# Scores of a whole tile as two matmuls in tiles of 64 rows by 128 columns of TensorE, in place of four in tiles of 64 by 64

## The chip, the cores and the metric

The kernel runs on one core of one Trainium2 chip. The metric is the device time of one execution in microseconds. Engines are named as in the profile: PE is TensorE (PEld its weight loads), DVE is VectorE, ACT is ScalarE, POOL is GpSimd, SP is SyncE, which issues the DMAs.

## What is computed

Attention over 4 batches, 8 heads, 576 positions and 64 values per head, where each query keeps its 32 largest scores; behind it two feed-forward stages on the 2304 x 512 result. All inputs and outputs are f32. The reference, cut:

```python
scores = scale * np.matmul(q, k.transpose(0, 1, 3, 2))          # 4 x 8 x 576 x 576
kth = np.partition(scores, -top_k, axis=-1)[..., -top_k:-top_k + 1]
scores = np.where(scores >= kth, scores, -1000000000.0)
attn = softmax of scores                                        # written out in the reference
attn_out = np.matmul(attn, v)                                   # -> x: 2304 x 512

h = x @ w_in                                                    # 512 -> 2048
x = (h * (1.0 / (1.0 + np.exp(-1.702 * h)))) @ w_out            # 2048 -> 512

h = (x @ w1) * (x @ w2) @ w3                                    # 512 -> 1024 -> 1024
out = h @ w_out2                                                # 1024 -> 512
```

## The kernel before

**Tiles and chunks.** The 2304 tokens are cut into eight chunks of 288 (`CHUNK`), two to a batch. A chunk has 18 tiles of attention work (`CT`): for each of two groups of four heads (`g`) there are eight whole tiles of 128 queries of one head (two parts `t.j` of four heads), and ahead of them one leftover tile (`t.left`) that holds the last 32 queries of the four heads, 4 x 32 = 128 rows. In all that is 144 tiles, 128 whole ones and 16 leftover ones. A tile is a matrix of 128 queries by 576 scores.

**One slot, one tile.** Each engine has its own program, all written as a list of slots, one for each tile, by `run_chunks` and a function `step`. The order within a slot is written out by hand. PE's slot (lines 750 to 774) has: `scores` of the tile two slots ahead (L616), `transpose_probs` of a tile four slots back (L630, five transposes of 128 x 128), then three or four feed-forward units of 12 matmuls each with 288 moving columns of f16 (L702), and, every other slot, `weigh_values` of a pair of tiles (L661). In the first slots PE also spreads peaks of the weights over the partitions (`spread_peaks`, L672, one to three matmuls with an f32 stationary operand of 128 x 128) and multiplies w3 by w_out2 (`weight_product`, L694).

**The scores.** `qx` holds the queries and `kx` the keys of a group, both transposed: 64 values of a head on the partitions. SP loads both a second time into the other 64 partitions (`both_halves`), so that partitions 0 to 63 work on the first 288 keys (`half` 0) and partitions 64 to 127 on the other 288 (`half` 1). The results of the two halves go to two banks of PSUM, `ps[:, half, 0:288]`. A matmul (line 616) takes 64 rows of the array, from row `half * 64` on, and as many columns as it has queries; `tile_position` says which. In a whole tile the 128 queries are taken in two parts of 64, which gives four matmuls in four tiles of 64 by 64 of the array. In a leftover tile the four heads have 32 queries each, which gives eight matmuls in tiles of 64 by 32. The last of them signals `qk_done`. Stationary is the slice of queries, moving are 288 columns of keys.

**What waits for the scores.** PE itself waits ahead of them for `s_copied`, ACT's copy of the tile before out of PSUM (L790), since there is one pair of banks. ACT copies the tile, DVE searches its 32 largest values (L975 to L995, seven passes over three slots), POOL scales the edges (L1199), ACT makes the penalty (L801), POOL subtracts it (L1191), ACT takes the exponentials (L810), DVE and POOL invert and apply the sum (L1003, L1216), and then come the transposes and ACT's copy of them (L819). The feed-forward units pass through ACT (tanh L864, g_high L877), DVE (gate L1010) and POOL (g_low L1227) meanwhile. At the end of each chunk DVE also finds a peak (L1097).

**The stretches.** Up to about 310 us DVE, ACT and POOL also read the weights, find their peaks and split them into two f16 parts; from there on the same 18 slots repeat for each chunk until 970 us, and behind 970 us only feed-forward work is left.

Of the kernel before, what the change touches and what calls it, by code (L numbers as in the profile page):

```python
# [12 lines left out]
B, H, S, D = 4, 8, 576, 64  # L13
TOKENS, DM, FF1, FF2 = B * S, H * D, 2048, 1024
TOP_K = 32
P = 128
# [4 lines left out]
HG = 4  # L21
# [216 lines left out]
def wait_alone(eng, sem, value, passed):  # L238


    wait(eng, sem, value)
    if not isinstance(value, int):
        eng.sem_inc(passed, 1)
# [19 lines left out]
def build(nc, q_in, k_in, v_in, w_in_d, w_out_d, w1_d, w2_d, w3t_d, wo2_d, out_d, wx_d, w3o_d):  # L263
# [160 lines left out]
    with nc.Block() as block:  # L424
# [171 lines left out]
        def _(pe):  # L596
            def scores(t):

                if not t.exists():
                    return  # L600
                if t.left:

                    pe.wait_ge(q_loaded[t.g], t.chunk.count(32, 32))
                    pe.wait_ge(k_loaded[t.g], t.chunk.batch_count(32, 32))

                wait_alone(pe, s_copied, t.count(), passed_pe)
                if t.left:
                    parts = [(i, slice(FULL, CHUNK), i * LEFT) for i in range(HG)]
                else:
                    first = t.j * P  # L610
                    parts = [(t.h % HG, slice(first + c, first + c + D), c) for c in (0, D)]
                for i, queries, col in parts:
                    for half in range(2):

                        rows = slice(half * D, (half + 1) * D)
                        last = nc.tensor.matmul(ps[col:col + queries.stop - queries.start, half, 0:HALF],  # L616
                                                qx[rows, t.g, i, queries],
                                                kx[rows, t.g, i, half * HALF:(half + 1) * HALF],
                                                start=True, stop=True, tile_position=(half * D, col))
                last.then_inc(qk_done, 1)  # L620
# [129 lines left out]
            def step(chunk):  # L750
                for slot in slots(chunk):
                    at = slot.at()
                    product = at - WPROD_FIRST if at is not None else -1
                    units = units_in(slot)
                    scores(slot.next(2))
                    transpose_probs(slot.next(-4))
                    if at == V_SCALE_SLOT:
                        spread_peaks(0, 1, 0)
                    if at == W_SCALE_SLOT:
                        spread_peaks(1, 2, slot.next(-6).group_count())  # L760
                    if at == SECOND_SCALE_SLOT:
                        spread_peaks(2, 3, slot.next(-6).group_count())
                    spread_for = period_at(slot, X2_SPREAD)
                    if spread_for is not None:
                        spread_x2(spread_for)
                    for u in units[:1]:
                        unit(u)
                    if 0 <= product < 2 * WBLK:
                        weight_product(2 * product)
                    for u in units[1:]:  # L770
                        unit(u)
                    if 0 <= product < 2 * WBLK:
                        weight_product(2 * product + 1)
                    weigh_values(slot.next(-4))
# [509 lines left out]
```

## Time and profile before

| | us |
|---|---|
| median of 3 runs | 1141.3 |
| lowest, highest | 1140.41, 1143.19 |
| the profiled execution | 1140.66 |
| its span, from the first to the last instruction | 1138.9 |
| PE busy | 1043.7 |
| DVE busy | 877.6 |
| ACT busy | 675.0 |
| POOL busy | 566.4 |

An f32 matmul stands in the trace as two records, and so does its weight load. Busy time counts an engine's time with at least one instruction under way; matmuls overlap, so their durations don't add up to it. The records of PE's matmuls have modelled ends: the distance of two starts says more than the end of one. Times of the timeline and of the chain count from the start of the span.

### The profile page before, as it was taken

What the parts mean: (1) busy time and instruction counts of PE and PEld (TensorE: products, weight loads), DVE (VectorE), ACT (ScalarE), POOL (GpSimd) and SP (SyncE); (2) the same over time, 40 slices, a digit from 0 to 9 for tenths busy, and PEclk for the clock granted to TensorE, in tenths of its full rate; (3) what the DMA queues carried; (4) which work ended last, traced back from release to release, by engine and by line L of the source; (5) the groups of instructions that cost most, each with busy time, mean ns of one, the idle gap of its engine ahead of it and who ended that gap; (6) DMA issues with size and microseconds to landing.
All of it is one profiled execution on the core that took longest, in us unless ns stands there. A gap on an engine that the chain in (4) does not pass through costs nothing.

```text
span 1138.9 us, 27527 instructions
## 1 busy us (share of the span) xinstructions
PE 1043.7 (92%) x9452; PEld 754.4 (66%) x9452; DVE 877.6 (77%) x1970; ACT 675.0 (59%) x1346; POOL 566.4 (50%) x806
## 2 busy tenths in 40 slices
PE   2499878697799999999999999999999999999989
PEld 0244456465577777777677767777777767887767
DVE  5999998987798789877998789978987899422010
ACT  2358888877866467645765576546755676444112
POOL 1334678876775346543654356534753475413001
PEclk9999989788999999999999999999999999999999
DMA  9963632574444051433032232503140304033144
GB/s 292 374 222 112 182 99 79 145 203 148 149 148 118 2 147 40 134 73 117 23 113 59 68 93 81 155 29 111 47 126 1 96 20 122 10 96 94 56 142 141
DMA packets 63471, 127.14 MB, mean 112 GB/s; under 512 B 5728, under 2 KB 22624, under 8 KB 61536
## 3 DMA queue, kind: packets, MB, share of 16 engines
q1 hardware_dynamic: 63328, 125.33, 37.3%
q8 instruction: 78, 1.28, 0.5%
q14 instruction: 65, 0.53, 0.2%
HBM read 112.20 MB, written 13.11 MB: 110 GB/s over the span
## 4 chain that ended last, share of the span: by engine, by line
PE 66%; DVE 12%; issue 8%; POOL 7%; ACT 4%; DMA 2%; SPq 1%; DVEq 0%; POOLq 0%; ACTq 0%
PE ff_ps L702 48%; PE x_T_ps L661 7%; PE probs_T_ps L630 6%; PE scores_ps L616 5%; DVE peaks L1026 2%; POOL scores L1191 2%; DMA v_three_quarters<-v_rows_in 2%; POOL g_low L1227 2%; DVE search L992 1%; DVE top L983 1%; DVE top L975 1%; DVE search L986 1%; DVE search L980 1%; POOL piece_split L1231 1%; POOL scores L1216 1%
## 5 line engine op out<-in xcount | busy, mean ns | idle before, releaser
L1191 POOL TENSOR_TENSOR scores<-scores,penalty 128x576 f32<-128x576 f32 x144 | 203.1, 1410 | 111.7 <-ACT penalty L801 111.6
L702 PE MATMUL ff_ps<-x_high,w_ring 128*128 128x288 f16 x1024 | 195.9, 288 | 3.8 <-DVE x_low L1124 3.8
L819 ACT ACTIVATE probs_T<-probs_T_ps 128x640 f32<-128x640 f32 x144 | 100.9, 700 | 109.3 <-PE probs_T_ps L630 108.6
L801 ACT ACTIVATE penalty<-scores,edges 128x576 f32<-128x576 f32 x144 | 111.2, 772 | 83.6 <-POOL edges L1199 81.6
L702 PE MATMUL ff_ps<-x_T_high,w_in_high 128*128 128x288 f16 x512 | 149.2, 291 | 10.6 <-DVE gate L1010 10.2
L702 PE MATMUL ff_ps<-x_T_low,w_in_high 128*128 128x288 f16 x512 | 148.9, 291 | 0.0
L702 PE MATMUL ff_ps<-x_T_high,w_in_low 128*128 128x288 f16 x512 | 148.7, 290 | 0.0
L702 PE MATMUL ff_ps<-g_high,w_out_high 128*128 128x288 f16 x512 | 147.6, 288 | 0.0
L702 PE MATMUL ff_ps<-g_low,w_out_high 128*128 128x288 f16 x512 | 147.5, 288 | 0.0
L702 PE MATMUL ff_ps<-g_high,w_out_low 128*128 128x288 f16 x512 | 147.5, 288 | 0.0
L702 PE MATMUL ff_ps<-x_low,w_ring 128*128 128x288 f16 x512 | 147.4, 288 | 0.0
L630 PEld LDWEIGHTS probs_T_ps<-identity,scores 128*128 128x128 f32 x720 | 79.5, 145 | 92.6 <-issue 52.2
L616 PE MATMUL scores_ps<-keys,queries 64*64 64x288 f32 (+1 forms) x1280 | 110.4, 452 | 32.9 <-ACT scores L790 18.6
L630 PE MATMUL probs_T_ps<-identity,scores 128*128 128x128 f32 x720 | 114.7, 292 | 26.4 <-POOL scores L1216 26.4
L1227 POOL TENSOR_TENSOR g_low<-gate,g_high 128x288 f16<-128x288 f32 x128 | 92.8, 732 | 71.2 <-ACT g_high L877 70.5
L661 PE MATMUL x_T_ps<-probs_T,v_rows 128*64 128x128 f32 (+1 forms) x1920 | 110.9, 267 | 14.2 <-ACT probs_T L819 6.9
L1216 POOL TENSOR_SCALAR scores<-scores,inverse_total 128x576 f32<-128x576 f32 x144 | 107.7, 748 | 31.8 <-DVE inverse_total L1003 31.7
L975 DVE MAX8 top<-scores 128x8 f32<-128x576 f32 x144 | 108.1, 751 | 15.8 <-ACT scores L790 13.8
L702 PEld LDWEIGHTS ff_ps<-x_high,w_ring 128*128 128x128 f16 x1024 | 100.6, 98 | 29.0 <-issue 3.9
L661 PEld LDWEIGHTS x_T_ps<-probs_T,v_rows 128*64 128x64 f32 x1920 | 93.5, 144 | 38.2 <-issue 38.2
L1227 POOL TENSOR_TENSOR ab_low<-gate,ab_high 128x288 f16<-128x288 f32 x64 | 46.8, 732 | 139.8 <-ACT ab_high L886 139.8
L810 ACT ACTIVATE scores<-scores,edges 128x576 f32<-128x576 f32 x144 | 111.4, 774 | 4.4 <-POOL scores L1191 4.1
(90 smaller groups left out, 2178.5 us busy)
## 6 DMA issues: line engine op xcount, KB each, us to landing
w_ring<-second_weights SPq DMA_DIRECT2D x192, 256.0 KB, 2.6
queries<-q_T SPq DMA_DIRECT2D x32, 288.0 KB, 4.5
keys<-k_T SPq DMA_DIRECT2D x16, 576.0 KB, 8.5
second_weights<-piece_split SPq DMA_DIRECT2D x24, 256.0 KB, 4.4
out<-y_out SPq DMA_DIRECT2D x32, 144.0 KB, 2.9
v_rows<-v_rows_in SPq DMA_DIRECT2D x8, 512.0 KB, 4.2
w_T<-w_T_in SPq DMA_DIRECT2D x1, 4096.0 KB, 39.9
whole_weight<-w_in SPq DMA_DIRECT2D x2, 2048.0 KB, 16.9
```

What stands on the lines that cost most here:

```text
L616: last = nc.tensor.matmul(ps[col:col + queries.stop - queries.start, half, 0:HALF], qx[rows, t.g, i, queries], kx[rows, t.g, i, half * HAL ...
L630: last = nc.tensor.transpose(ptp[:, j * P:(j + 1) * P], row[:, min(j * P, S - P):min((j + 1) * P, S)], ident[:, :])
L661: last = nc.tensor.matmul(xq[odd * D:(odd + 1) * D, cols], vn[:, j, first:first + D], pt[:, tile.ring(2), j * P + queries.start:j * P + qu ...
L702: last = nc.tensor.matmul(out, stationary[i], moving[j], start=first and n == 0, stop=last_one and n == 2)
L801: act.activation(pen[:, :], sc[:, t.ring(RING), :], ACT.Relu, bias=thr[:, r:r + 1], scale=-PENALTY).then_inc(pen_done, 1)
L810: act.activation(row, row, ACT.Exp, bias=negm[:, r:r + 1], scale=SCALE, accum_out=total[:, r:r + 1]).then_inc(exp_done, 1)
L819: act.activation(pt[:, t.ring(2), :], ptp[:, 0:PADDED], ACT.Copy).then_inc(pt_copied, 1)
L975: nc.vector.max(tops[:, 0:8], row).then_inc(search_a, 1)
L1026: nc.vector.tensor_reduce(peaks[:, i:i + 1], src, AXIS.X, ALU.max, apply_absolute_value=True).then_inc(found, 1)
L1191: pool.tensor_tensor(row, row, pen[:, :], ALU.subtract).then_inc(masked_done, 1)
L1216: pool.tensor_scalar(row, row, rinv[:, r:r + 1], 1.0, ALU.mult, ALU.mult).then_inc(norm_done, 1)
L1227: pool.tensor_tensor(low, gf[:, u.ring, :], high, ALU.subtract).then_inc(signal, 1)
```

## The change

A whole tile's list of parts has one entry in place of two: all 128 queries of the tile's head, from column 0. The loop below it is unchanged, and makes one matmul for each half of the keys, with a stationary operand of 64 x 128, at rows 0 and 64 of the array and column 0. `D` is 64 and `P` is 128. The leftover tiles, the operands in SBUF, the results in PSUM, and all signals and waits are as before.

```diff
                 if t.left:
                     parts = [(i, slice(FULL, CHUNK), i * LEFT) for i in range(HG)]
                 else:
-                    first = t.j * P
-                    parts = [(t.h % HG, slice(first + c, first + c + D), c) for c in (0, D)]
+                    parts = [(t.h % HG, slice(t.j * P, (t.j + 1) * P), 0)]
                 for i, queries, col in parts:
                     for half in range(2):
```

## Rows read from the trace of the kernel before

**Rows 1.** The page: span, and busy us (share of the span) of engines.

```profile
span 1138.9 us, 27527 instructions
PE 1043.7 (92%) x9452; PEld 754.4 (66%) x9452; DVE 877.6 (77%) x1970; ACT 675.0 (59%) x1346; POOL 566.4 (50%) x806
```

**Rows 2.** Busy time of each engine by stretch: length, then busy us (instructions), clock, DMA.

```profile
175.00:238.00 63.00, 47.26 (x403) 31.97 (x395) 56.51 (x140) 54.59 (x94) 52.13 (x61) 0.78 0.43 114
...
366.00:426.00 60.00, 60.00 (x591) 45.04 (x587) 48.06 (x111) 33.61 (x68) 25.34 (x41) 1.00 0.27 68
426.00:487.00 61.00, 59.98 (x583) 44.47 (x581) 56.55 (x130) 41.05 (x89) 38.38 (x57) 1.00 0.34 96
```

**Rows 3.** Waits of PE from 320 to 970 us: total us, times, longest.

```profile
PE ff_ps L702 <- DVE gate L1010: 5.1, 10, 0.8
```

**Rows 4.** Waits of PE from 0 to 320 us.

```profile
PE probs_T_ps L630 <- POOL scores L1216: 26.4, 17, 4.0
PE scores_ps L616 <- ACT scores L790: 18.6, 9, 6.4
```

**Rows 5.** Chain of waits, 424 to 449 and 526 to 562 us: start, us, what.

```profile
426.08 0.64 PE scores_ps L616 x16
...
440.19 0.65 PE scores_ps L616 x8
...
526.82 0.65 PE scores_ps L616 x8
...
560.93 0.65 PE scores_ps L616 x8
```

**Rows 6.** Chain of waits, 155 to 260 us: first and last whole-tile step.

```profile
159.94 1.17 PE scores_ps L616 x8
...
257.48 0.64 PE scores_ps L616 x8
```

**Rows 7.** Groups by line and shape on PE, 310 to 970 us, then 0 to 310.

```profile
L616 PE MATMUL scores_ps<-keys,queries 64*64 64x288 f32 x696 | 62.3, 428 | 2.5 <-issue 2.5
...
L616 PE MATMUL scores_ps<-keys,queries 64*64 64x288 f32 x328 | 36.1, 518 | 18.7 <-ACT scores L790 18.6
```

**Rows 8.** Timeline of PE, 600.5 to 601.5 us: start, us, instruction (a whole tile).

```profile
600.58 0.29 PE L702 MATMUL ff_ps<-x_high,w_ring 128*128 128x288 f16 x1
600.79 0.21 PEld L616 LDWEIGHTS scores_ps<-keys,queries 64*64 64x64 f32 x8 [0.24 <-issue]
...
601.09 0.42 PE L616 MATMUL scores_ps<-keys,queries 64*64 64x288 f32 x4
601.44 0.14 PEld L630 LDWEIGHTS probs_T_ps<-identity,scores 128*128 128x128 f32 x1 [0.44 <-issue]
```

**Rows 9.** Timeline of PE, 607.7 to 608.5 us (a leftover tile).

```profile
607.79 0.43 PE L616 MATMUL scores_ps<-keys,queries 64*32 64x288 f32 x1
...
608.05 0.45 PE L616 MATMUL scores_ps<-keys,queries 64*32 64x288 f32 x8
608.43 0.14 PEld L630 LDWEIGHTS probs_T_ps<-identity,scores 128*128 128x128 f32 x1 [0.46 <-issue]
```

**Rows 10.** Durations by line, ns, least/median/most, over short stretches.

```profile
L616 PE MATMUL scores_ps<-keys,queries x8: 402/428/454, 600.8 to 601.1; 64*64 64x288 f32 x8
...
L616 PE MATMUL scores_ps<-keys,queries x16: 402/414/428, 607.8 to 608.1; 64*32 64x288 f32 x16
...
L672 PEld LDWEIGHTS x_T_ps<-peak_diagonal,ones x4: 186/190/193, 108.6 to 109.0; 128*128 128x128 f32 x4
L672 PE MATMUL x_T_ps<-peak_diagonal,ones x4: 275/275/377, 108.6 to 109.1; 128*128 128x128 f32 x4
...
L630 PE MATMUL probs_T_ps<-identity,scores x5: 272/273/328, 601.4 to 601.9; 128*128 128x128 f32 x5
...
L702 PEld LDWEIGHTS ff_ps<-x_high,w_ring x3: 98/98/98, 600.1 to 600.5; 128*128 128x128 f16 x3
```

## The prediction, made before the change was run

> **What bounds the kernel now.** I read the page's shares first, then the stretches by time, then who PE waited for, then the chain of waits. The page has PE busy for 92% of the span, DVE for 77% [rows 1]. That is a mean over two regimes, and the stretches part them. From about 310 us on PE is busy 60.0 us of 60.0 and 59.98 of 61.0, at the full clock [rows 2]; in the 650 us from 320 to 970 it waits for DVE 5.1 us in all, in ten pieces [rows 3]. There a nanosecond more on PE is a nanosecond more of span, nearly. Before 310 us it is the other way: DVE, ACT and POOL also prepare the weights, PE waits for POOL 26.4 us and for ACT's copies of the scores 18.6 us [rows 4], and the clock granted is 0.78 in the worst stretch [rows 2]. There a longer PE instruction mostly eats into a wait.
>
> PE's program goes slot by slot: scores of the tile two slots ahead (L616), transposes of an older tile (L630), three or four feed-forward units (L702), every other slot the value product (L661). So the scores lie between matmuls of other shapes, and what counts is how long PE is held from the last matmul before them to the first one after.
>
> **The change part by part.** One tile's 128 queries now go as two matmuls, 64 rows by 128 columns, where they went as four, 64 by 64. Each f32 matmul shows as two records, two passes, so 8 records become 4 in each of the 128 whole tiles (1024 records, 696 of them after 310 us, 328 before) [rows 7]. The 16 leftover tiles (64 by 32) stay as they are. Operands, results, semaphores, DMAs and the work of the other engines stay too; nothing is moved and no wait is added.
>
> *How a score step is built up today.* The last L702 matmul starts at 600.58; matmuls of that kind follow each other by 0.12, so its columns are through at 600.70, and the scores start at 600.79: 0.09 us go at the change of shape. The four first passes start nearly together, the second passes at 601.09, the transposes at 601.44; the step is 0.65 us [rows 8]. The four tiles therefore run side by side, and the time is that of one tile: a first load, two passes, a stagger between the tiles, and again a change of shape.
>
> - The load. Before the first pass the weights must come in, and the record of the first pass contains that: 454 ns against 402 for a second pass, so 52 ns for 64 columns. With 32 columns it is 428 against 402, 26 ns. With 128 columns of f32, on the spread of the peaks (L672), 377 against 275, 102 ns [rows 10]. It follows the columns of the stationary operand, not its rows: 26, 52, 102.
> - The passes. From the first pass to the second are 0.30 us with 64 columns [rows 8] and 0.26 with 32 [rows 9]. Less the loads of 52 and 26 ns, that leaves 0.24 us for 288 moving columns in either shape. Two passes are 0.48. The change keeps 288 moving columns and two passes; with half as many tiles in flight nothing is gained, since they ran side by side.
> - The stagger. The four second passes together take 0.42 us where one takes 402 ns, so the last starts 18 ns behind the first, 6 for each [rows 8, 10]; with eight tiles 0.45 against 402, 48 ns [rows 9, 10]. Two tiles: 6 ns.
> - The rest, 0.65 - 0.052 - 0.48 - 0.018 = 0.10 us, is the change of shape behind the step. The leftover step checks the construction: 0.026 + 0.48 + 0.048 + 0.10 = 0.65, measured 608.43 - 607.79 = 0.64 [rows 9].
>
> The new step: 0.102 (load, from the 128-column row) + 0.48 + 0.006 + 0.10 = 0.69 us. Load and stagger were 52 + 18 = 70 ns and become 102 + 6 = 108, **38 ns more** for each whole tile. I take the L672 row for the load, since it is f32, no transpose and 128 columns. The nearest rows on the low side are the transposes, also 128 columns of f32: 328 against 273, 55 ns exposed. And an f16 load of 128 columns takes 98 ns where the f32 one takes 190, 92 less, which would leave 10 ns exposed [rows 10]. On the high side the load of the second pass could come out of cover too, another 102 ns. Today the eight loads of a step are over 0.21 us after its start, inside the first pass [rows 8], and I leave that so: two loads of 102 ns end at 0.20, the first pass at 0.34.
>
> A rule of the Trainium skill speaks against this change here. The page TensorE: Matmul & The Clock Gate (Part 3, The mechanism) says that a weight load overlaps a running matmul only where its row group is another. By that rule the second pass's load would wait for the first pass, and the sum would be 38 + 102 = 140 ns a tile. The trace does not bear it out: the second loads lie under first passes that occupy both row groups [rows 8].
>
> *How many of these 38 ns reach the end.* Of 696 / 8 = 87 whole-tile steps after 310 us, 13 are off the chain. In four places it leaves PE as at 526.82 and comes back at 560.93, through DVE, POOL and ACT, past three whole-tile steps and one leftover one; and once between 426.08 and 440.19, past one [rows 5]. There the extra 0.04 to 0.11 us are covered by PE's own wait for DVE, about 1 us each time (5.1 us in five places) [rows 3]; if that cover were gone they would cost 13 x 0.038 = 0.5 us. The other 74 count: 2.8 us. Of the 41 steps before 310 us (328 / 8), five are on the chain, the first at 159.94, the last at 257.48 [rows 6]: 0.2 us. The other 36 delay scores that lie in front of the search in a stretch where PE waits anyway [rows 4]; nothing is charged, and 36 x 0.038 = 1.4 us would be the cost without cover. Behind 970 us there are no scores.
>
> Sum: 79 x 0.038 = **3.0 us**. The profiled execution has a span of 1138.9 in 1140.66 us, 0.6 below the median of 1141.3. Its span would be 1141.9, its time 1143.7; put to the median, **1144.3 us**, 0.26% more. A comparison of this kernel can tell some 0.3%, 3.4 us, from no change, so this is just inside.
>
> **The rivals.**
> 1. *The cover is gone* (slower). The load costs as forecast, but the start-up and the thirteen covered steps pay too, as the late scores reach the copy, the search and the penalty in turn. It decides from the point where more than 90 of the 128 steps pay, 90 x 0.038 = 3.4. All: 128 x 0.038 = 4.9 us, 1146.2. For it: ACT's copies and DVE's search follow the scores. Against it: PE waits over 45 us for others in the start-up [rows 4].
> 2. *The second load in the open* (slower): 79 x 0.140 = 11.1 us, 1152.4. Against it: today's second loads are hidden [rows 8]. The page's rule named above gives this same case.
> 3. *The two tiles of rows don't run side by side* (slower): two more passes of 0.24, so 0.48 + 0.038 us a tile, 79 x 0.518 = 41 us, 1182. Against it: of today's four, two share their columns and differ in rows, and all start within 18 ns.
> 4. *A shorter load.* At the transposes' 55 ns the tile has 55 + 6 - 70 = -9 ns, -0.7 us, 1140.6: same. At the 10 ns left by an f16 load, -54 ns, -4.3 us, 1137.0: faster. For the second the trace has nothing but f16, and the f32 load of 128 columns stands at 190 ns. The Trainium skill's page TensorEngine Tiling (Gotcha 2) says that column tiling excludes the fast weight load; leaving column tiling, as here, could be read as letting it in, with this second price. No f32 row shows such a load.
> 5. *The change of shape goes* (faster). If only a division of the columns makes PE run empty, 64 by 128 needs neither of the 0.09 and 0.10 us, and the load hides under the matmuls ahead: 0.65 + 0.09 - 0.49 = 0.25 us less a tile, up to 79 x 0.25 = 20 us. DVE is busy 56.5 us of 61 in every other stretch [rows 2] and would hold back part; I take 15, 1126. No row shows a change of rows alone, so only likeness to the changes seen speaks against it.
> 6. *The start-up falls otherwise.* 22% of 63 us below full clock is 28 us at the half level [rows 2]; what a shift of PE's waits does to it has no row. The three runs differ by 2.8 us; I take that to either side.
>
> **How the numbers follow.** The forecast has 0.70. Since 3.0 lies 0.4 under the bound and runs scatter by more, I give 0.44 of it to same and 0.26 to slower. Rival 1 has 0.08 (slower), 2 has 0.03 (slower), 3 has 0.02 (slower), 4 has 0.03 (same) and 0.04 (faster), 5 has 0.06 (faster), 6 has 0.04 (half faster, half slower). Faster 0.12, same 0.47, slower 0.41. The range goes from 1139.5, below the shorter load of the transposes' kind, to 1147.0, above the case without cover with 0.8 for scatter; outside lie the fast load, 2, 3, 5 and most of 6, about 0.18.
>
> **What would show it.** In the profile after: 512 score records of 64 by 128; first passes of 402 + 102, about 504 ns, second ones of 402; loads of about 190; 0.34 from first to second pass (rival 2: 0.44; rival 3: the second tile's pass a further 0.24 behind); 0.69 from the scores to the transposes; 0.09 ahead of them still (rival 5: none). One period of two chunks, 560.93 - 440.19 = 120.74 us today [rows 5], longer by 28 steps at 38 ns, 1.1 us, but for what PE's waits absorb. The forecast is wrong if the load isn't 102, if these steps are longer and the period isn't, or if the start-up to 310 us moves by more than a microsecond.

## The result, and the profile after

| | before | after |
|---|---|---|
| median | 1140.39 us (20 runs, 1137.07 to 1143.61) | 1144.86 us (20 runs, 1143.39 to 1147.19) |
| ratio | | 1.0037, 95% interval 1.0029 to 1.0044 |

The change costs 4.2 us (3.3 to 5.0); measured again on another occasion, the ratio was 1.0040 (1.0024 to 1.0056). Forecast were 3.0 us, 0.26%, and a time of 1144.3. The sign held, and the time lies within the stated range. The measured 4.2 us are above the bound of 3.4 us that the prediction put between same and slower, so it came out as slower (0.41) and not as same (0.47). That 1144.3 and 1144.86 lie close is partly luck: the median before was 1140.39 here, 0.9 below the 1141.3 from which the forecast counted. The difference is the measure, 4.2 against 3.0.

The profiled execution of the changed kernel is, with 1147.19 us, the slowest of its 20, so its span is not used as the measure. Its page, to be held against [rows 1]:

```profile
span 1145.4 us, 26503 instructions
PE 1052.4 (92%) x8940; PEld 769.0 (67%) x8940; DVE 878.2 (77%) x1970; ACT 675.6 (59%) x1346; POOL 566.1 (49%) x806
```

There are 512 matmuls and 512 weight loads fewer, and PE is busy longer (1045.4 us in before_again, 1052.1 in after_again). DVE, ACT and POOL have as many instructions as before, and their busy times differ by 0.6 us at most.

The step itself, in the timeline of the changed kernel (start, us, instruction), answers to [rows 8]:

```profile
603.94 0.29 PE L701 MATMUL ff_ps<-x_high,w_ring 128*128 128x288 f16 x1
604.15 0.30 PEld L615 LDWEIGHTS scores_ps<-keys,queries 64*128 64x128 f32 x4 [0.24 <-issue]
...
604.50 0.41 PE L615 MATMUL scores_ps<-keys,queries 64*128 64x288 f32 x2
604.84 0.14 PEld L629 LDWEIGHTS probs_T_ps<-identity,scores 128*128 128x128 f32 x1 [0.39 <-issue]
```

Durations in that step, ns, least/median/most, against [rows 10]:

```profile
L615 PEld LDWEIGHTS scores_ps<-keys,queries x4: 182/184/186, 604.2 to 604.3; 64*128 64x128 f32 x4
L615 PE MATMUL scores_ps<-keys,queries x4: 402/455/507, 604.2 to 604.5; 64*128 64x288 f32 x4
```

These rows bear out the construction of the prediction nearly term by term. A first pass takes 507 ns against 402 for a second one: 105 ns of load in the open, where 64 columns had 52. The second passes start 0.35 us after the first ones, where it was 0.30. The transposes start 0.69 us after the scores, where it was 0.65. Ahead of the scores 604.15 - 603.94 = 0.21 us pass, as between 600.58 and 600.79 before, so the change of shape still costs its 0.09.

PE's waits for DVE from 320 to 970 us are 4.9 us, against 5.1 [rows 3]:

```profile
PE ff_ps L701 <- DVE gate L1009: 4.9, 10, 0.7
```

The best ruler for the stretch behind 310 us is the start of one instruction that comes once in a chunk, the spread of the peak of x2. In the timelines of PE, before and then after:

```profile
420.04 0.28 PE L683 MATMUL x_T_ps<-peak_diagonal,ones 128*128 128x128 f32 x1
...
540.78 0.28 PE L683 MATMUL x_T_ps<-peak_diagonal,ones 128*128 128x128 f32 x1
...
661.54 0.28 PE L683 MATMUL x_T_ps<-peak_diagonal,ones 128*128 128x128 f32 x1
...
784.70 0.28 PE L683 MATMUL x_T_ps<-peak_diagonal,ones 128*128 128x128 f32 x1
```

```profile
422.62 0.28 PE L682 MATMUL x_T_ps<-peak_diagonal,ones 128*128 128x128 f32 x1
...
543.94 0.28 PE L682 MATMUL x_T_ps<-peak_diagonal,ones 128*128 128x128 f32 x1
...
665.26 0.28 PE L682 MATMUL x_T_ps<-peak_diagonal,ones 128*128 128x128 f32 x1
...
789.19 0.28 PE L682 MATMUL x_T_ps<-peak_diagonal,ones 128*128 128x128 f32 x1
```

One chunk with its 16 whole tiles lasts 120.75 us before (241.50 over two) and 121.32 after (242.64 over two): 0.57 us more, 0.036 for each whole tile. The chunk with the edge of the loop in it is longer in both, 123.16 and 123.93; more of that below.

### The profile page after: what moved, and what is told of

Read it like the earlier page. It is cut to its first block, busy times and chain, and to the rows that moved or that the text cites. A ratio compares the mean times of both kernels' runs of the same rounds, so it can differ in the third digit from the quotient of the medians.

```text
span 1145.4 us, 26503 instructions
## 1 busy us (share of the span) xinstructions
PE 1052.4 (92%) x8940; PEld 769.0 (67%) x8940; DVE 878.2 (77%) x1970; ACT 675.6 (59%) x1346; POOL 566.1 (49%) x806
## 3 DMA queue, kind: packets, MB, share of 16 engines
q1 hardware_dynamic: 63328, 125.33, 37.2%
## 4 chain that ended last, share of the span: by engine, by line
PE 66%; DVE 11%; issue 8%; POOL 7%; DMA 4%; ACT 3%; SPq 1%; DVEq 0%; POOLq 0%; ACTq 0%
PE ff_ps L701 47%; PE x_T_ps L660 7%; PE probs_T_ps L629 6%; PE scores_ps L615 5%; DVE peaks L1025 2%; DMA v_three_quarters<-v_rows_in 2%; DMA second_weights<-piece_split 2%; POOL scores L1190 2%; DVE search L991 1%; POOL piece_split L1230 1%; PE ff_ps L693 1%; POOL g_low L1226 1%; DVE top L982 1%; DVE search L985 1%; DVE top L974 1%
## 5 line engine op out<-in xcount | busy, mean ns | idle before, releaser
L615 PE MATMUL scores_ps<-keys,queries 64*128 64x288 f32 (+1 forms) x768 | 116.5, 469 | 34.1 <-ACT scores L789 19.6
L974 DVE MAX8 top<-scores 128x8 f32<-128x576 f32 x144 | 108.2, 752 | 15.7 <-ACT scores L789 13.9
```

The lines of the kernel that those rows point to most:

```text
L974: nc.vector.max(tops[:, 0:8], row).then_inc(search_a, 1)
```

## The experiments

Kernels that ran together share their runs of the kernel before. The theory is that of the prediction: the wider first load stands in the open behind a change of shape, PE is the bound behind 310 us, and others cover it ahead of that.

### Where in the program the time arises

`e1_startup_only` has the change in the first two chunks, `e2_rest_only` in the other six.

```diff
-                    parts = [(t.h % HG, slice(first + c, first + c + D), c) for c in (0, D)]
+                    width = P if t.chunk.reg is None and t.chunk.off < 2 else D      # e1
+                    width = P if t.chunk.reg is not None or t.chunk.off >= 2 else D  # e2
+                    parts = [(t.h % HG, slice(first + c, first + c + width), c) for c in range(0, P, width)]
```

> The 64 by 128 tiles in the whole tiles of the first two chunks alone (32 of the 128), which run before about 300 us. The profile of the changed kernel shows the step 0.04 us longer (0.69 against 0.65). Theory of the prediction: PE waits for others there, five of these steps lie on the chain, so +0.2 us. Rival (the cover is gone): all pay, 32 x 0.04 = +1.3 us, which would make up the difference between the 3.0 us forecast and the 4.2 us measured.

> The 64 by 128 tiles in the whole tiles of the other six chunks alone (96 of 128). Theory of the prediction: 74 of them on the chain with 0.04 us, +3.0 us. If the covered ones pay too: 96 x 0.04 = +3.9 us. If the cost came mainly from the start-up: under +2 us.

Measured: e1 1.0005 (0.9995 to 1.0014), that is +0.6 us (-0.6 to 1.6). e2 1.0039 (1.0025 to 1.0053), +4.4 us (2.9 to 6.0). Most of the cost sits behind the first two chunks; the start-up's part is too small for this comparison and can't be told between 0.2 and 1.3 us. e2's interval holds both 3.0 and 3.9.

To make the start-up's part visible, `e10_startup_three_pieces` lengthens the same 32 steps by five times as much. It combines e1 with the edit of e6 below.

```diff
+                    early = t.chunk.reg is None and t.chunk.off < 2
+                    width = P if early else D
...
+                    pieces = 3 if not t.left and early else 1
```

> The kernel before, but in the first two chunks alone whole tiles have 64 by 128 tiles with three pieces of 96 moving columns, which lengthens the step by 0.197 us (0.843 against 0.646 in the trace of e6), five times what the change does. Theory of the prediction (five of the 32 lie on the chain): +1.0 us. If the start-up has no cover: 32 x 0.197 = +6.3 us.

Measured: 1.0026 (1.0012 to 1.0040), +3.0 us (1.4 to 4.6). It is between the two, and its interval holds neither: 3.0 / 0.197 is as much as 15 of the 32 steps at 0.197 us, 7 to 23 by the interval. The five steps on the chain of one execution [rows 6] were too few. At 15 steps the change's own 0.041 us makes 0.6 us in the start-up; e1's 0.6 agrees, but its interval holds 0.2 as well.

The count is rough, for not every step has the price of 0.197 us there. Early in the start-up the step of the kernel before lasts 1.16 us, as in the first row of [rows 6], and not 0.65. From PE's timelines, the start of the ninth step and of the transposes behind it, before, in the changed kernel and in e10:

```profile
51.47 0.76 PE L616 MATMUL scores_ps<-keys,queries 64*64 64x288 f32 x4 [1.33 <-ACT scores L790]
...
52.63 0.47 PE L630 MATMUL probs_T_ps<-identity,scores 128*128 128x128 f32 x1
```

```profile
52.82 0.85 PE L615 MATMUL scores_ps<-keys,queries 64*128 64x288 f32 x2 [1.33 <-ACT scores L789]
...
54.08 0.48 PE L629 MATMUL probs_T_ps<-identity,scores 128*128 128x128 f32 x1
```

```profile
53.08 0.53 PE L620 MATMUL scores_ps<-keys,queries 64*128 64x96 f32 x2 [1.34 <-ACT scores L794]
...
54.60 0.47 PE L634 MATMUL probs_T_ps<-identity,scores 128*128 128x128 f32 x1
```

Such a step is 0.10 us longer with the change and 0.36 in e10, a quarter or so. If such steps carry the cost, 3.0 us in e10 stand for 0.8 us of the change, so 0.6 to 0.8 is the estimate. Which steps pay was not shown. A single profile can't show it: the first spread of the peak of x2 starts at 297.43 us in e10 and at 293.84 in e6, which has the same steps in the start-up, and at 292.27 and 293.65 in the two profiles of the kernel before.

### What sets the length of the step

`after_again` is the changed kernel; beside it three kernels run that cut the 288 moving columns of a whole tile's matmuls into pieces. Each piece has a weight load of its own, so that a load meets a shorter pass.

```diff
-                    for half in range(2):
+                    pieces = 1 if t.left else 2          # e5; 3 in e6 and e7
+                    piece = HALF // pieces
+                    for half, p in [(half, p) for p in range(pieces) for half in range(2)]:
 
                         rows = slice(half * D, (half + 1) * D)
-                        last = nc.tensor.matmul(ps[col:col + queries.stop - queries.start, half, 0:HALF],
+                        last = nc.tensor.matmul(ps[col:col + queries.stop - queries.start, half, p * piece:(p + 1) * piece],
                                                 qx[rows, t.g, i, queries],
-                                                kx[rows, t.g, i, half * HALF:(half + 1) * HALF],
+                                                kx[rows, t.g, i, half * HALF + p * piece:half * HALF + (p + 1) * piece],
```

In e5 and e6 this stands on the changed kernel, in e7 on the kernel before, with the pieces as the outermost loop.

> The changed kernel again, beside the others of this call. By the first measurement +0.37%, 4.2 us, against the forecast of 3.0.

> The changed kernel with the 288 moving columns of each matmul of a whole tile in two pieces of 144, the two tiles of rows in turn: a load of 102 to 107 ns for each pass of 120 ns. Theory (each load but the first lies under the pass ahead): nothing more than the changed kernel, step 0.69 to 0.71 us. If loads of one row group waited for the running matmul: 3 loads more in the open, 0.3 us a tile, +25 us.

> The same in three pieces of 96: passes of 80 ns are shorter than the load of 107 ns. Theory: the loads now set the pace, six of 107 and a last pass of 80: step 0.107 x 6 + 0.08 + 0.10 = 0.82 us against 0.65 before, +0.17 us a tile, some +14 to 16 us against before. If the load were only a fixed cost ahead of the first pass: as the changed kernel, +4 us.

> The kernel before, whole tiles in four tiles of 64 by 64, with the moving columns in three pieces of 96. The load of 64 columns, 53 ns, is shorter than the pass of 80 ns. Theory: it stays hidden, step 0.65 to 0.68 us, within 2 us of before. If the count of instructions were the cost (24 records where 8 were): a step as long as with 128 columns, +14 us.

The timelines of PE show the steps, from the first load of the scores to that of the transposes. e5:

```profile
601.77 0.55 PEld L617 LDWEIGHTS scores_ps<-keys,queries 64*128 64x128 f32 x8 [0.24 <-issue]
601.77 0.76 PE L617 MATMUL scores_ps<-keys,queries 64*128 64x144 f32 x8
602.46 0.14 PEld L631 LDWEIGHTS probs_T_ps<-identity,scores 128*128 128x128 f32 x1
```

e6:

```profile
602.25 0.91 PE L617 MATMUL scores_ps<-keys,queries 64*128 64x96 f32 x12
...
603.09 0.20 PEld L631 LDWEIGHTS probs_T_ps<-identity,scores 128*128 128x128 f32 x2
```

e7:

```profile
604.61 0.73 PE L618 MATMUL scores_ps<-keys,queries 64*64 64x96 f32 x24
605.27 0.14 PEld L632 LDWEIGHTS probs_T_ps<-identity,scores 128*128 128x128 f32 x1
```

| kernel | columns of a load | moving columns of a pass | step, expected, us | step, measured, us | ratio to before |
|---|---|---|---|---|---|
| after_again | 128 | 288 | 0.69 | 0.69 | 1.0040 (1.0024 to 1.0056) |
| e5 | 128 | 144 | 0.69 to 0.71 | 0.69 | 1.0031 (1.0019 to 1.0044) |
| e6 | 128 | 96 | 0.82 | 0.84 | 1.0149 (1.0125 to 1.0172) |
| e7 | 64 | 96 | 0.65 to 0.68 | 0.66 | 1.0059 (1.0039 to 1.0080) |

e5 has four loads for each tile of rows and pays for one, as the changed kernel does. Its three later loads run under a pass on the same rows of the array, and the step is 691 ns where it was 687. So the sentence of the Trainium skill that the prediction weighed (TensorE: Matmul & The Clock Gate, Part 3, a load overlaps only where the row group is another) does not hold here; by it three loads of 0.105 us would have come into the open, 0.3 us a tile.

e6 shows the other side. Where a pass streams for 240 x 96 / 288 = 80 ns and the load needs some 105, the load sets the pace, and the step grows by 0.15 us over the changed kernel. e7 has the same short passes and twice as many instructions as e6, with loads of half the columns, and its step grows by 0.01 us alone. It is the columns of the stationary operand that count, not the number of instructions.

e6 is also a second gauge for the share that reaches the end. Its ruler in the timeline:

```profile
547.19 0.28 PE L684 MATMUL x_T_ps<-peak_diagonal,ones 128*128 128x128 f32 x1
...
670.70 0.28 PE L684 MATMUL x_T_ps<-peak_diagonal,ones 128*128 128x128 f32 x1
```

A chunk lasts 123.51 us, 2.76 more than before; 2.76 / 0.197 = 14.0 of the 16 steps. For the changed kernel the lengthening is 507 - 454 = 53 ns of load less 12 ns of stagger (two tiles fewer at 6 each), 0.041 us, and 0.57 / 0.041 = 13.9. Two costs that differ fivefold give the same count. The two steps that don't pay are absorbed where PE waits for DVE. The trace shows one of them directly: PE's waits from 320 to 970 us shrink from 5.1 us before to 4.9 after and 4.1 in e6, in five chunks, about 0.2 each in e6:

```profile
PE ff_ps L703 <- DVE gate L1011: 4.1, 10, 0.6
```

The whole comes out in the main: 87 steps behind 310 us x 14/16 x 0.197 = 15.0 us, and 3.0 in the first two chunks (e10), 18.0 together, where e6 measured 17.0 (14.3 to 19.6). Between the two lie nine steps of the third chunk (41 before 310 us, 32 of them in the first two); if all of them pay, 1.8 us come on top, and 19.8 is just outside.

e7 is a miss in its time: expected within 2 us of before, measured +6.7 (4.5 to 9.1), though step and chunk (120.91 us, the distance of the same spreads at 544.54 and 665.45) are as expected. What the other microseconds are is taken up with e3.

### Less load, more stagger

`e3_columns_32` takes a whole tile as eight matmuls in tiles of 64 by 32, like a leftover tile.

```diff
-                    parts = [(t.h % HG, slice(first + c, first + c + D), c) for c in (0, D)]
+                    parts = [(t.h % HG, slice(first + c, first + c + LEFT), c) for c in range(0, P, LEFT)]
```

> Whole tiles as eight matmuls in tiles of 64 rows by 32 columns, as the leftover tiles are. Theory (first load by columns, then a stagger of 6 ns for each further tile): load 26 and stagger 45 ns in place of 52 and 18, the step stays 0.65 us and the time the same as before within 0.5 us. If the number of instructions were what costs (the change has fewer and is slower, so this is the opposite): 16 records more a tile, faster than before. If only the load counted: 0.026 us x 79 = 2 us faster.

The step was as expected, 0.65 us (646 ns), and the chunk with it, 120.76 us, the same as before:

```profile
540.84 0.28 PE L683 MATMUL x_T_ps<-peak_diagonal,ones 128*128 128x128 f32 x1
...
661.60 0.28 PE L683 MATMUL x_T_ps<-peak_diagonal,ones 128*128 128x128 f32 x1
...
790.12 0.28 PE L683 MATMUL x_T_ps<-peak_diagonal,ones 128*128 128x128 f32 x1
```

Yet the kernel was slower than the one before, 1.0037 (1.0024 to 1.0050), +4.3 us, against the expectation. The third row shows where most of it lies: the chunk from 661.60 to 790.12 lasts 128.52 us, 5.36 more than in the profile of before. It holds the edge at which the loop over pairs of chunks starts over. The timeline of PE in e3 there, with the wait ahead in brackets:

```profile
684.65 0.70 PE L616 MATMUL scores_ps<-keys,queries 64*32 64x288 f32 x3 [2.91 <-issue]
687.61 1.21 PE L616 MATMUL scores_ps<-keys,queries 64*32 64x288 f32 x13 [2.25 <-issue]
```

PE stands still for 2.91 and again for 2.25 us, in the midst of the scores and for nothing that the profile shows. In the kernel before it is one such wait of 2.5 us. Then the clock falls. Busy time, clock and DMA from 676 to 700 us (as in [rows 2]), for before, the changed kernel and e3:

```profile
676.00:700.00 24.00, 20.46 (x192) 15.06 (x191) 21.71 (x53) 16.13 (x39) 16.02 (x23) 1.00 0.15 38
```

```profile
676.00:700.00 24.00, 20.35 (x168) 14.94 (x167) 22.09 (x48) 16.59 (x39) 15.80 (x23) 1.00 0.04 11
```

```profile
676.00:700.00 24.00, 17.83 (x152) 12.05 (x151) 17.29 (x42) 13.58 (x32) 12.13 (x18) 0.86 0.02 5
```

A mean clock of 0.86 in 24 us is 6.7 us at the half level, 1.2 GHz, behind the wait. The comparison of e3 with before is therefore no test of the step's length; its trace is.

`before_again` shows how far this edge moves by itself.

> The kernel before against itself. Every theory: ratio 1.000 within its interval; the trace shows whether the period of one chunk (120.75 us), the 2.5 us PE stands at the edge of the loop near 684 us, and the stretches at half clock repeat.

Measured: 1.0004 (0.9989 to 1.0019), same times. Its chunk repeats to 0.01 us (540.90 to 661.65), but not the edge: there PE stood 3.1 us, and the clock is 0.93 in place of 1.00:

```profile
676.00:700.00 24.00, 19.92 (x167) 14.39 (x166) 20.48 (x49) 15.75 (x37) 14.59 (x22) 0.93 0.09 23
```

The same program loses another 2.2 us here (661.65 to 786.98 is 125.33 against 123.16). So of e3's 5.36 us at the edge only 3.2 stand against a kernel before that lost as well; that is inside the 2.7 to 5.7 measured. The other kernels with the loop agree: over an ordinary chunk of its own, the chunk with the edge is longer by 4.6 us in before_again and by 4.3 to 4.6 in e1, e2, e8 and e10. It is longer by only 2.4 in the profile of before, and by 2.6 and 2.7 in those of the changed kernel.

For e7, where the chunk with the edge lasts 126.52 us, it is 1.2 us against before_again, and its other chunks add 0.16 each, 0.9 in all; some 4.5 us remain of its 6.7. Its profile has 3.3 of them in the first 60 us, where PE waits 18.4 us for ACT's copies and 15.1 in before_again. The trace shows where that comes from. ACT's copy waits in turn for POOL and DVE, and DVE for a DMA that brings three quarters of v; it lands 3.1 us later in e7 than in before_again, though it was issued at 5.2 and 5.1 us. DVE's timelines, e7 and then before_again:

```profile
27.41 2.55 DVE L1028 TENSOR_REDUCE peaks<-v_three_quarters 128x1 f32<-128x2304 f32 x1 [3.51 <-DMA v_three_quarters<-v_rows_in]
```

```profile
24.30 2.55 DVE L1026 TENSOR_REDUCE peaks<-v_three_quarters 128x1 f32<-128x2304 f32 x1 [0.21 <-DMA v_three_quarters<-v_rows_in]
```

That is no cost of the scores. It is one profile against one, and whether e7 has this in its other executions is not known, so 4.5 us of its time stay unexplained. A single profile can't tell such a loss from an effect of a change, and a difference of 2 us between two spans says nothing on the scores.

### The order of the steps

If a change of shape and the load behind it are what costs, the order of the steps in a slot has a price. The transposes have the shape of the feed-forward matmuls, so that nothing is lost between those two.

```diff
-                    scores(slot.next(2))
-                    transpose_probs(slot.next(-4))
+                    transpose_probs(slot.next(-4))
+                    scores(slot.next(2))
```

> The kernel before with the transposes ahead of the scores in every slot of PE. Theory (a load stands in the open only behind a change of shape, and by its own columns): where no value product lies ahead, the transposes' load of 55 ns goes under the feed-forward matmuls and the first f16 load behind the scores is exposed in its place, some 10 to 25 ns: 30 to 45 ns less in half of the slots, some 1.5 to 2 us faster. Rival: the scores come 0.6 us later for ACT and the search, which gives it back in the stretches where DVE is the bound: same or slower by up to 3 us.

Measured: 1.0014 (1.0003 to 1.0025), slower by 1.6 us, and a chunk of 120.87 us (542.11 to 662.98), 0.12 more. The rival said slower, but the reason is another: I had looked at the slots without a value product alone. PE's wait for DVE didn't grow: from 320 to 970 us it is 2.2 us in e4, where it was 5.1, so DVE doesn't explain the longer chunk. (Ahead of 310 us the rival isn't excluded.) Where `weigh_values` ends the slot before, the order L661, L630, L616, L702 changes shape once more than L661, L616, L630, L702. `e8_mixed_order` therefore changes the order only where no value product lies ahead.

```diff
+                    after_values = slot.next(-5).exists() and slot.next(-5).ends_group()
+                    if after_values:
+                        scores(slot.next(2))
                     transpose_probs(slot.next(-4))
+                    if not after_values:
+                        scores(slot.next(2))
```

> The kernel before with the transposes ahead of the scores only in slots without a value product right ahead of them (4 of 9 slots); in the others the scores stay first. In the trace of e4 such a slot spends 1.41 us from the last feed-forward matmul to the first one after both steps, against 1.46 before, while a slot with a value product loses 0.10 through a fourth change of shape. Theory (a change of shape and the load behind it are the cost): 64 x 0.055 = 3.5 us less if all count, some 2.5 us less for those after 310 us. Rival: scores that come later cost DVE more than that: same or slower.

The chunk is now 120.54 us (538.49 to 659.03), 0.21 less than before, half of what was expected (8 x 0.055 = 0.44). The time can't be told from that of before: 0.9997 (0.9983 to 1.0011). The sign of the reason is right in the trace; its worth of some 1 us is too small for the comparison of times, and the missing half was not searched for.

`e9_mixed_unrolled` also writes out all chunks, and with that takes away the edge of the loop.

```diff
-    for c in range(4):
-        step(Chunk(c))
-    with eng.Fori(0, (NCHUNK - 4) // 2) as i:
-        step(Chunk(4, i))
-        step(Chunk(5, i))
-    step(Chunk(NCHUNK))
-    step(Chunk(NCHUNK + 1))
-    step(Chunk(NCHUNK + 2))
+    for c in range(NCHUNK + 3):
+        step(Chunk(c))
```

> e8 with all chunks written out in place of the loop over pairs of chunks (all engines). Before, PE stands 2.5 us at the edge of the loop, and in some traces the clock falls to half for 3.4 to 6.8 us behind it. Theory: both go, and with them what register arithmetic costs DVE and POOL: 2.5 to 5 us less than e8. Rival: the longer program makes the fetch of instructions wait elsewhere: nothing gained.

Measured: 0.9968 (0.9954 to 0.9981), 3.7 us faster than before (2.2 to 5.3) and 2.9 us below e8's median beside it. e9's chunk over the place of the edge has the length of every other, 120.54 us:

```profile
662.90 0.38 PE L677 MATMUL x_T_ps<-peak_diagonal,ones 128*128 128x128 f32 x1
...
783.44 0.38 PE L677 MATMUL x_T_ps<-peak_diagonal,ones 128*128 128x128 f32 x1
```

This version beats both kernels. The change studied here has no part in it.

## Why the prediction was right, and where not

**The step.** Right in all its terms at full clock. Forecast 0.102 + 0.48 + 0.006 + 0.10, 38 ns more; the trace gives 105 for the load, passes and change of shape as they were, and 41 in all. The row of another instruction (L672) with the same number of columns and the same type gave the price of a load that the kernel before did not have in the scores, to 3 ns. That two tiles of rows run side by side, that the second load stays hidden, and that the change of shape stays, all came as forecast; rivals 2, 3 and 5 and both prices of rival 4 are excluded by the rows of after. The transposes' 55 ns for a load of as many columns, the low neighbour in the prediction, stay without an explanation.

**The share behind 310 us.** Forecast 74 of 87 steps; measured by two costs of different size 14 of 16, that is 76. 76 x 0.041 = 3.1 us in place of 2.8. Steps off the chain were covered, as forecast, though 11 and not 13 of them: PE's wait for DVE shrank from 5.1 to 4.9 us. There was a slip in the part on what would show it: the stretch of 120.74 us is one chunk with 16 whole tiles, not two chunks with 32, and the expected 28 steps and 1.1 us should have read 14 and 0.5 us. Measured were 0.57. The sum did not rest on it, since it counted the steps by the records.

**The start-up.** This is the term that was mis-sized. Forecast 5 of 41 steps and 0.2 us, because the chain of waits of one execution passes five of them; e10's 3.0 us are worth about 15 of 32 steps (7 to 23), 0.6 to 0.8 us for the change. The prediction also put 38 ns on every step, though its [rows 6] has one of 1.17 us, and such a step grew by some 0.10. The nine steps of the third chunk ahead of 310 us, which e10 leaves as they were, cost at most 9 x 0.041 = 0.4 us more; no run prices them. The likely reason for the count is that the chain names only the path that ended last in one execution, and that a step off it can have less slack than the delay put on it; no experiment tests that by itself. Rival 1, that all pay, would be 6.3 us or more in e10 and is excluded in the start-up by its 4.6, behind 310 us by the 14 of 16. Rival 6, that the clock of the start-up falls otherwise, left no mark in the profiles: from 0 to 310 us the mean granted clock is 0.93 and 0.92 in the two of before and 0.92 in both of after.

**The sum.** 3.1 + 0.6 = 3.7 us, and 3.1 + 0.8 + 0.4 = 4.3 with the dearer steps and the third chunk; both are inside the measured 3.3 to 5.0. The 0.7 or more above the forecast carried the time over the bound of 3.4 us, 0.3 of it behind 310 us and the rest ahead. With a point 0.4 us under the bound and the cover as the least certain term, near-even chances for same and slower were a fair statement.

**What stays open.** The middle of the measurement is 4.2, and the sum is 3.7 to 4.3. It is an average over executions, while the edge of the loop alone differs by 2.2 us between two profiles of one kernel, so the agreement is no closer than that. All three profiles of kernels that have 64 by 128 everywhere with one or two pieces (after, after_again, e5) show a longer time at the half level behind 1098 us, clock 0.76 in 14 us where before has 0.88:

```profile
1098.00:1112.00 14.00, 13.03 (x93) 9.86 (x94) 2.20 (x4) 2.64 (x7) 1.46 (x2) 0.88 0.46 137
```

```profile
1098.00:1112.00 14.00, 10.21 (x61) 6.96 (x59) 2.75 (x7) 2.33 (x4) 0.00 (x0) 0.76 0.45 130
```

From the last spread to the end of the span are 45.3 us after (from 1100.10) and 44.1 before (from 1094.80). If this belongs to the change, the sum lacks about a microsecond. The other kernels with the wide tiles in part or in three pieces (e1, e2, e6) don't show it. Whether it belongs to the change or to where a wait of PE happens to fall was not settled.

## What to carry to other kernels

Behind a change of tile shape the first weight load of the scores stood in the open, and its price went by the columns of the stationary operand (26, 52, 105 ns for 32, 64, 128), though the transposes' load of 128 columns cost 55: fewer and wider matmuls can be slower than more and narrower ones that run side by side. Price such an edit by a row of another instruction with the same columns and type, count the steps by the records, and gauge the share that pays by doubling or quintupling the cost rather than by the chain of one execution. For a difference under half a percent use the distance of an instruction that recurs once in each round; it repeated to 0.01 us here, where whole executions of one program differ by 6 us.

## What was not expected of the hardware

- At the edge of the loop PE stood 2.5 to 3.1 us in the kernel before, for nothing that the profile shows, and 2.9 and 2.3 us in two pieces in e3. More instructions alone don't make the second piece: e7, with 24 records for a whole tile where e3 has 16, has one wait of 3.0. In some profiles the clock fell to the half level behind it for 3 to 7 us (0.93 and 0.86 of 24 us), in others not. With the chunks written out (e9) the profile has neither at this place.
- Weight loads of the same rows of the array ran under a matmul as long as they were shorter than it: 105 ns under 120 ns (e5) cost nothing, 105 under 80 (e6) made the step 0.15 us longer, where five further loads that each outlast their pass by 25 ns would make 0.13; and 53 under 80 (e7) made it 0.01 longer.
